# A recurrent-attention and two-MLP kernel on one core: its issue tables set anew, with instruction packets counted as transfers

## What is computed

```python
for t in range(S):
    y[:, :, t] = einsum('bhd,bhde->bhe', r_t, state + u*k_t v_t)
    state = w_t[..., None] * state + k_t v_t
# x: (3072, 384), the heads side by side
h = x @ w_in                       # (3072, 1024)
sm = exp(h - max(h)) / (sum + 1e-9)
ln = layernorm(h * sm) * g_ln
x = ln @ w_out                     # (3072, 384)
g = relu(x @ w2_in) ** 2           # (3072, 2048)
return g @ w2_out                  # (3072, 384)
```

## Time and profile before

| what | value |
|---|---|
| median of 3 runs | 809.27 us (807.33 to 810.18) |
| the profiled execution, its own time | 809.33 us |
| its span, first to last instruction | 807.6 us |
| PE busy, of the span | 754.4 us (93%) |
| DVE, ACT, POOL busy | 62%, 55%, 19% |
| DMA engines, mean share; data moved | 45%; 125.5 MB |
| granted TensorE clock, mean | 0.984 |

### The profile page before, as it was taken

How to read it: one execution, slowest core, us unless ns; L and a number is a source line. 1 busy time by engine, 2 the same in 40 slices (tenths; PEclk the granted TensorE clock), 3 DMA queues, 4 the chain that set the end, 5 groups by cost and what they waited for, 6 DMA issues and landing times.

```text
span 807.6 us, 25806 instructions
## 1 busy us (share of the span) xinstructions
PE 754.4 (93%) x10624; PEld 639.2 (79%) x10624; DVE 497.6 (62%) x1079; ACT 441.1 (55%) x966; POOL 151.2 (19%) x241
## 2 busy tenths in 40 slices
PE   2668979999979999999999999999999999999997
PEld 1457869878878888888888888888788888888886
DVE  7685976976646855737854737855565862543333
ACT  5684875864645755654655555664563673333222
POOL 4332220330221212210321210320310210000000
PEclk9988999999989999999999999999999999999999
DMA  7424575376355235355235255235344233344652
GB/s 236 151 67 155 187 255 169 123 241 222 118 198 181 95 135 204 101 176 196 93 135 200 86 196 191 97 133 176 111 158 140 93 136 104 137 163 150 215 194 100
DMA packets 34021, 125.54 MB, mean 155 GB/s; under 512 B 5104, under 2 KB 10608, under 8 KB 33904
## 3 DMA queue, kind: packets, MB, share of 16 engines
q1 hardware_dynamic: 33712, 123.79, 44.7%
q10 hardware_dynamic: 192, 0.10, 0.0%
HBM read 105.39 MB, written 17.30 MB: 152 GB/s over the span
## 4 chain that ended last, share of the span: by engine, by line
PE 87%; issue 4%; DVE 4%; ACT 3%; DMA 1%; SPq 1%; POOL 0%; DVEq 0%; ACTq 0%; POOLq 0%
PE acc L664 24%; PE hid L649 24%; PE flex L632 13%; PE flex L601 12%; PE flex L531 4%; PE flex L615 3%; PE flex L571 2%; PE flex L558 2%; PE flex L546 1%; ACT att L1031 1%; PE flex L582 1%; PE flex L510 1%; PE flex L535 1%; DMA o_stage<-in_win 1%; DVE att L776 1%
## 5 line engine op out<-in xcount | busy, mean ns | idle before, releaser
L649 PE MATMUL hid<-y_hi,w 128*128 128x512 f32 (+1 forms) x624 | 203.0, 383 | 0.8 <-issue 0.7
L664 PE MATMUL acc<-g_hi,w 128*128 128x512 f32 (+1 forms) x624 | 200.7, 381 | 1.7 <-DVE g_lo L897 1.2
L893 DVE TENSOR_TENSOR act<-act 128x512 f32<-128x512 f32 (+1 forms) x104 | 70.1, 674 | 116.0 <-ACT g_hi L1031 116.0
L1258 POOL TENSOR_TENSOR k_t<-k_t,w_up 128x256 f32<-128x256 f32 x120 | 82.3, 701 | 315.4 <-PE flex L531 262.9
L649 PEld LDWEIGHTS hid<-y_hi,w 128*128 128x128 f32 x624 | 117.4, 192 | 23.2 <-issue 1.3
L664 PEld LDWEIGHTS acc<-g_hi,w 128*128 128x128 f32 x624 | 114.8, 188 | 24.6 <-issue 1.7
L649 PE MATMUL hid<-y_lo,w 128*128 128x512 f32 (+1 forms) x312 | 118.0, 378 | 0.0
L664 PE MATMUL acc<-g_lo,w 128*128 128x512 f32 (+1 forms) x312 | 116.9, 375 | 0.0
L1031 ACT ACTIVATE act<-hid 128x512 f32<-128x512 f32 (+1 forms) x104 | 58.6, 563 | 103.7 <-PE hid L649 102.9
L1031 ACT ACTIVATE r_right<-r_t 64x256 f32<-64x256 f32 x240 | 100.0, 417 | 27.7 <-DVE r_t L808 25.2
L632 PE MATMUL flex<-ln_hi,out_hi 128*128 128x256 f32 x288 | 81.3, 282 | 0.5 <-DVE ln_lo L877 0.5
(11 more groups left out here) (107 smaller groups left out, 1151.1 us busy)
## 6 DMA issues: line engine op xcount, KB each, us to landing
w<-split_w SPq DMA_DIRECT2D x88, 768.0 KB, 4.5
split_w<-w SPq DMA_DIRECT2D x16, 768.0 KB, 5.3
r_t<-in_rT SPq DMA_DIRECT2D x11, 512.0 KB, 5.1
k_t<-in_kT SPq DMA_DIRECT2D x11, 512.0 KB, 5.0
w_t<-in_wT SPq DMA_DIRECT2D x11, 512.0 KB, 6.7
v_n<-in_vN SPq DMA_DIRECT2D x12, 384.0 KB, 5.2
out<-o_stage SPq DMA_DIRECT2D x5, 768.0 KB, 7.1
o_stage<-in_w2in SPq DMA_DIRECT2D x16, 192.0 KB, 2.9
```

What stands on the lines that cost most here:

```text
L649: last = mm(hid[:, cols], w2[:, step % RING, w, k * P:(k + 1) * P], y[:, k, cols], start=n == 0, stop=n == len(terms) - 1)
L664: last = mm(acc[:, d, cols], w2[:, step % RING, w, rows], gx[:, step % 2, cols], start=j == 0 and n == 0, stop=j == final and n == 2, skip ...
L893: e.tensor_tensor(act[:, step % 2, cols], act[:, step % 2, cols], act[:, step % 2, cols], ALU.mult).then_inc(g_ready, 1)
L1258: e.tensor_tensor(halves(k_t[K_BUF[l + 1]][:, half(h)], l)[:, :, 0, :], left, right_w, ALU.mult).then_inc(k_ready[h], 1)
```

## The change

No instruction is added, removed or resized: every engine has the same instructions before and after, 297 transfers on SP among them. The five tables are replaced as a whole; their numbers come from a planner outside the kernel, which now also counts the packets that carry TensorE's own instructions as transfers that queue behind the data. Two rows of the SP table and one of the PE table, as they read in the diff:

```diff
 SP_AT = [
...
-    {"load_w": 9, "load_odd": 6, "load_k": 12, "repack": 16, "load_r": 13, "load_v": 17, "keep": {9: 2, 11: 4, 10: 5, 13: 8, 12: 11, 14: 14}, "load":
-     {11: 0, 12: 1, 13: 3, 14: 7, 15: 10, 16: 15}},
...
+    {"load_w": 15, "load_odd": 7, "load_k": 14, "repack": 16, "load_r": 4, "load_v": 13, "keep": {9: 0, 10: 6, 13: 9, 14: 10, 11: 11, 12: 17}, "load":
+     {11: 1, 12: 2, 13: 3, 14: 5, 15: 8, 16: 12}},
...
```

More of the change, by code:

```diff
@@ L57 @@
[L57 to L61, removed]
+    {"load_w": 2, "load_odd": 6, "load_k": 1, "repack": 7, "load_r": 5, "load_v": 9, "load": {5: 0, 6: 3, 7: 4, 8: 8}},
@@ L64 @@
 PE_AT = [
[L65 to L69, removed]
+    {"level": ((1, 2), (6, 4), (7, 9), (8, 11), (10, 13), (12, 14)), "bonus": (0, 3), "k_natural": 15, "output": 16, "state": 17, "read_state": 5},
@@ new lines @@
+    {"level": ((3, 0), (4, 7), (12, 10), (13, 11), (16, 14), (17, 15)), "bonus": (2, 8), "k_natural": 18, "output": 21, "state": 23, "read_state": 20,
+     "hidden1": ((1, 5), (6, 9)), "ln": (19, 22), "narrow": (24, 25, 26)},
+    {"level": ((0, 8), (7, 10), (14, 15), (17, 16), (22, 24), (23, 26)), "bonus": (3, 11), "k_natural": 31, "output": 34, "state": 37, "read_state":
+     33, "hidden1": ((1, 9), (20, 21)), "ln": (29, 35), "narrow": (38, 39, 40), "up": (2, 4, 6, 13, 19, 27, 30, 36), "down": (-1, 5, 12, 18, 25, 28,
@@ L83 @@
+    {"level": ((5, 1), (6, 3), (10, 9), (12, 11), (22, 20), (23, 21)), "bonus": (0, 4), "k_natural": 31, "output": 34, "state": 42, "read_state": 33,
+     "hidden1": ((7, 8), (16, 17)), "ln": (27, 35), "narrow": (38, 39, 40), "up": (2, 13, 15, 19, 26, 29, 32, 37), "down": (14, 18, 24, 25, 28, 30,
+     36, 41)},
 ]
 DVE_AT = [
-    {"bonus": (0, 1), "carry": ((2, 3), (5, 6), (8, 10), (11, 14), (19, 20), (24, 25)), "w_products": 4, "scores": ((9, 16), (12, 18), (15, 21), (17,
-     23), (22, 26)), "output": 30, "state": 32, "x_low": 33, "piece": {0: 7, 1: 13, 2: 27, 3: 28, 4: 29, 5: 31}},
@@ L124 @@
-    {"side": ((2, 3), (7, 8), (18, 15)), "right": ((1, 0), (5, 4), (6, 10), (19, 13), (20, 16)), "place": (24, 25), "level5": (29, 26), "k_natural":
-     31, "output": 33, "x_high": 37, "exp": (11, 21), "squares": (14, 23), "ln_high": (28, 32), "narrow": (34, 38, 39), "relu": (9, 12, 17, 22, 27,
-     30, 35, 36), "y_high": 40},
+    {"side": ((0, 4), (11, 12), (17, 20)), "right": ((1, 2), (6, 7), (8, 13), (14, 16), (18, 19)), "place": (21, 23), "level5": (22, 24), "k_natural":
+     25, "output": 27, "x_high": 29, "repack": 28, "piece": {0: 3, 1: 5, 2: 9, 3: 10, 4: 15, 5: 26}},
@@ new lines @@
+    {"side": ((0, 4), (10, 13), (17, 16)), "right": ((3, 2), (7, 5), (11, 8), (14, 12), (20, 15)), "place": (22, 21), "level5": (23, 24), "k_natural":
+     26, "output": 29, "x_high": 34, "exp": (9, 18), "squares": (19, 25), "ln_high": (27, 30), "narrow": (33, 35, 36), "y_high": 37, "repack": 32,
+     "piece": {6: 1, 7: 6, 8: 28, 9: 31}},
+    {"side": ((0, 9), (15, 13), (25, 22)), "right": ((5, 3), (8, 10), (12, 16), (20, 19), (24, 26)), "place": (28, 31), "level5": (30, 34),
+     "k_natural": 36, "output": 39, "x_high": 44, "exp": (14, 29), "squares": (23, 33), "ln_high": (37, 40), "narrow": (41, 43, 45), "relu": (2, 4,
+     11, 17, 21, 32, 35, 42), "y_high": 46, "piece": {10: 1, 11: 6, 12: 7, 13: 18, 14: 27, 15: 38}},
```

110 lines of the change are left out of this document (54 added, 56 removed).

## The result

The changed kernel takes 801.05 us (median of 4, 800.02 to 802.63) against 808.47 us of the kernel before on the same chip: ratio 0.9908, 95% interval 0.9881 to 0.9935, 7.4 us less. The forecast was 793, 16 less. So direction and range held, and under half of the size came. On a second chip the changed kernel gave 0.9933 (0.9905 to 0.9961).

What follows compares the result with a forecast made beforehand. PE's own work bounds it, plus opening chains and late instruction packets with low clock after. 809.33 - 9.3 (gaps) - 6.4 (clock) - 3.6 (shorter breaks) + 0.3 (left at place 1) + 2.9 (new waits) = 793.2; forecast 793, range 786 to 803.

Steps and rivals of the forecast that it cites:

- Place 1: Turn 2, unit 2's output: less data ahead of the packet cuts the 3.38 us break to 0.3; 1.7 clock returns.
- Place 3: Turn 9, inside hidden1: store and w no longer ahead of the packet, so 1.97 us break and 1.7 clock return.
- Place 2: Turn 4, unit 4's output: only one slice ahead of the packet, so 3.94 us break and 3.0 clock return.
- The seven breaks: Sign: PE's three large and four shorter issue breaks, 13.2 us together, come down to under 4.
- The shorter breaks: Four issue breaks of 0.88, 1.07, 1.09 and 0.85 us, sum 3.9; 3.6 forecast to return, 1.5 to 3.9 possible.
- New waits: PE waits added by the new order, including 0.5 us for packets at the starts of turns 5 and 7; sum 2.9.
- (a): Start of turn 2: PE's down waits for ReLU and g_lo behind two half-width up; 0.8 us, 0 to 1.5.
- (b): Odd repeated turns: only one up covers ln_lo before narrow1; 0.2 us x 4 = 0.8, from 0 to 2.
- (c): Turn 4 score behind a row maximum on DVE; turn 2 hidden1 needing ACT's narrow1 copy; 0.8 together, 0 to 1.5.
- Loads that go later: Delayed k, w and repack, and r for turn 1, still arrive before their use; cost nothing.
- Half comes back: Rival, 801 us, chance 0.18: opening waits for DVE instead, or packets late elsewhere in turns 1 to 5.
- The repeated turn loses its cover: Rival, 815 us, chance 0.05: store delays repack, ACT stands at x_high, PE's third narrow1 waits, four times over.

Runs made afterwards that it cites:

- e4: Kernel before, with 127 more already-reached semaphore waits at the start of PE's stream, order unchanged; 804.4 us, ratio 0.9966.
- e7: Changed kernel with 127 more already-reached semaphore waits at the start of PE's stream; 806.2 us, ratio 0.9990.
- e8: Changed kernel with 64 more already-reached semaphore waits at the start of PE's stream; 798.4 us, ratio 0.9906.
- e9: Kernel before, with each slice load of the second MLP's weights moving 8 KB instead of 768 KB (result wrong); 796.1 us, ratio 0.9850.
- e6: Kernel before with only the changed SP table (order of transfers), other engines in old order; 813.9 us, ratio 1.0081.
- e5: Changed kernel run again word for word, on a second chip; 801.6 us, ratio 0.9933 to the kernel before.
- e12: Changed kernel with the rows of the repeated turns (5 and 6) of all five tables put back as before; 804.4 us, ratio 0.9964.
- e3: Changed kernel with SP holding back the load of slice 23 until unit 4's read of the old state; 799.8 us, ratio 0.9907.
- e10: Changed kernel with slice loads of 8 KB instead of 768 KB (result wrong); 799.7 us, ratio 0.9896.
- e14: Changed kernel with 8 KB slices and SP's row of turn 4 alone put back as before; 799.0 us, ratio 0.9894.
- e13: Changed kernel with 8 KB slices and PE's row of turn 4 alone put back as before; 800.5 us, ratio 0.9914.

## Why the prediction was right and wrong, step by step

- **What bounds the kernel; the breaks are late packets of instructions.** Right, now shown by moving them with idle instructions (e4, e7, e8) and, in turns 4 and 9, by taking the data away (e9).
- **Place 1.** Right: 0.46 us left for a forecast of 0.3, the clock stayed at 1.00, the turn 4.3 us shorter for 3.6. That the transfers take the break away is shown by e6, though there PE's waits for ACT took the turn's gain. The 0.46 is chance in part: 1.46 in e5, whose turn 2 is 3.3 us shorter.
- **Place 3.** Right: 3.7 us for 3.67, undone by e12, and gone with small slices in e9.
- **Place 2.** The step that failed: "When the packet is asked for, only one slice of 768 KB stands ahead of it [...]: 3.94 us gone." The price was right (e9: 7.7 us for the whole of turn 4, 7.8 forecast), its return was mis-sized: 1.0 of 3.94 came. I took the moment of the request from the kernel before, as one block of 256 ahead, and looked only at what SP's new order put in front of it. In the new order the packet came later: 1.3 us of the 2.92 is a slice that went out in between (e3), 1.6 stays with the DMA engines idle ahead of the packet (e3) and with slices of 8 KB (e10). It isn't SP's row (e14); whether it is PE's isn't shown (e13), and why it comes late stays open. In this execution the clock was not given back either: the breaks of 2.14 and 2.92 us have each 3.4 us at 0.50 behind them, together the 6.8 that the one of 3.94 us had. In e5 and e12 half and all of it came back, and turn 4 paid 3.1 and 4.6 us of the 7.3.
- **The seven breaks, 13.2 us, to come under 4.** Three of them are left and a new one has come: 0.46 + 2.14 + 2.92 + 2.35 = 7.9 us. Of the signs named, PE's waits after 240 us and the start of turn 2 came out right; of the three `output` blocks only unit 3's is in one piece, and the clock is low twice after 100 us. **The shorter breaks, 3.6 back**, are the second term that failed. The one at 202.45, 0.85 us, became 2.14 with a low clock (none in e5); a new one of 2.35 opened in turn 0. In this execution the smaller breaks gave back about nothing in sum. A break under 1 us was read as a small cost; it is a packet with no slack, and another order can make it long.
- **New waits, 2.9.** Right in sum, not in kind. Waits for other engines from 80 us on are 5.0 us in the rows above, against 2.7 before (0.6 for k_flat, 0.4 for stats, 0.3 for g_lo and the two of the earlier trace rows): +2.3. (a) 0.3 for 0.8. (b) none for 0.8: no wait at L632 in the repeated turns. (c) 0.2 for 0.8, one of the two waits for DVE's `att`. (d) none for 0.5. Unforeseen: 1.2 us for DVE's state at the start of turn 3, and in turns 2 and 4 waits of 0.3 for ACT's `att` and `act` and 1.0 for stats (0.4 before).
- **Loads that go later, at nothing.** Right in the changed kernel, but for the opening, where no experiment took the loads apart. e6 shows what the cover is worth: without the other tables' new order PE waits 4.9 us for k_t and 2.4 us for `narrow1`'s copy.
- **Rivals.** "Half comes back (801)" is what happened, and by its second mechanism: packets late elsewhere in turns 1 to 5 and a middle break with its clock left. That it fits to the microsecond is luck: it had one middle break and 1 us more of new waits than the forecast, where there were three breaks of 2.1 to 2.9 us and 0.6 us less of waits, and a second execution, e5, has its time in other places. It had 0.18; its argument, that transfers are as dense as before in turns 1 to 5, deserved more weight than the order at the three largest places. "The repeated turn loses its cover" did not happen in the changed kernel. e6 has the first half of it: the `repack` late and ACT behind it at `x_high`; but PE then waits for ACT's copies of k at the start of the next turn, not in `narrow1`.

## What to carry to other kernels

In a long straight stream an "issue" break inside a run of equal instructions is a late block of instructions: count 256 instructions back, and look at what the DMA queues hold there. To be sure that it is one, move it (e4): the "issue" wait at 54.5 us did not move. Its cost is the break and often a stretch of low clock, and both can be taken away by reordering transfers, here only together with the engines that use them. When you price the return, don't take the moment of the request from the old order: it can move with the new one; look at more than one execution before you say that a turn gained nothing; and try the cheapest edit first, a few idle instructions at a place where the engine waits anyway, since it moves all blocks at once, at several distances, since here 32 and 64 waits won and 96 and 127 lost it again.

## What the runs showed of the hardware that I had not expected

- A packet can be late with idle DMA engines: it came 3.7 us after PE had entered the block before in the changed kernel (21.7 us), 4.4 in e10 (226.3) and 4.6 in e3 (226.8), but about when PE entered it in e9 (221.4). The Trainium skill, page "Runtime: NRT & Kernel Launch", section "Instruction fetch mechanics", has fetching hidden since the sequencer dispatches more slowly than blocks are filled; here neither kernel's trace agrees. What the request waits for stays open.
- PE goes on some 1.2 to 1.6 us after its packet has landed: in unit 4's break of the changed kernel the packet ended at 230.7 and PE went on at 231.9.
- Two semaphore waits in a row take one instruction: 64 of them added 32 instructions to PE's stream and moved the cut by 16 matmuls.
- The length of a break at the same place varies by 1 to 2 us between executions (unit 2's: 0.46 and 1.46). How much of the scatter of this kernel comes from it isn't shown.
- The low clock is no fixed price. Behind the breaks of 2.14 and 2.92 us it was 0.50 for 3.4 us, behind 0.46, 1.57 (e10) and 2.35 it stayed at 1.00; but behind the same break in turn 9 it fell in the kernel before (1.97 us) and not in e12 (1.99 us), and behind unit 4's break it did not fall in e12 either, with PE's next 4 us at 1.00:

```profile
232.08 0.66 PE L571 MATMUL flex<-att,v_n 64*48 64x64 f32 x30 [2.94 <-issue]
...
232.00:236.00 4.00, 3.92 (x58) 3.84 (x59) 1.99 (x4) 2.37 (x5) 1.04 (x2) 1.00 0.03 8
```
